# Attention, routing and two feed-forward layers in one kernel: the third batch's routing moved a round forward, and the steps at the hand-over reordered

## The reference

```python
def _attn_ref(q, k, v, alpha):           # 4 batches, 8 heads, 768 steps, head size 48
    for t in range(S):
        state = alpha[:, :, t, :, None] * state + np.einsum('bhd,bhe->bhde', k[:, :, t], v[:, :, t])
        y[:, :, t] = np.einsum('bhd,bhde->bhe', q[:, :, t], state)
def _moe_ref(x, expert_emb, tau, w1, w2):    # x: 3072 tokens of 384, 8 experts, hidden size 1024
    xn = x / (np.linalg.norm(x, axis=-1, keepdims=True) + 1e-06)
    logits = xn @ en.T / tau                 # en: the embeddings, normed alike
    expert_idx = np.argmax(logits, axis=1)
    gate_w = probs[np.arange(N), expert_idx] # probs: softmax of the logits
    for e in range(E):
        h = np.maximum(x[mask] @ w1[e], 0.0)
        out[mask] = gate_w[mask, None] * (h @ w2[e])
def _moe2_ref(x, w_in, w_out):               # hidden size 2048
    h = x @ w_in
    g = np.where(h > 0.0, h, np.exp(np.minimum(h, 0.0)) - 1.0)
    return g @ w_out
```

## Time and profile before

| | |
|---|---|
| median of 3 runs | 923.85 us (922.24 to 924.01) |
| the profiled execution | 922.87 us |
| its span | 921.2 us |
| PE busy | 886.1 us, 96% of the span |
| DVE busy | 435.5 us, 47% |
| ACT busy | 321.7 us, 35% |
| POOL busy | 273.0 us, 30% |
| mean granted clock of PE | 0.987 |

### The profile page before, as it was taken

The page is one execution under the profiler, slowest core; times in us unless marked ns, Lnnn a source line. Parts: engine busy times, 40 slices in busy tenths (PEclk is TensorE's granted clock), DMA queues, the critical chain, the costliest instruction groups (busy, mean ns, idle before and its releaser), DMA issues. The chain is left out here.

```text
span 921.2 us, 16309 instructions
## 1 busy us (share of the span) xinstructions
PE 886.1 (96%) x5729; PEld 779.3 (85%) x5729; DVE 435.5 (47%) x837; ACT 321.7 (35%) x708; POOL 273.0 (30%) x277
## 2 busy tenths in 40 slices
PE   7999999968999999999998999999999999999995
PEld 4777788757989899898997899999999999989994
DVE  6788787863222322223224545445445445445442
ACT  3556656622222222223222223223233223323221
POOL 2212444643576555635816400101001001001001
PEclk8999999979999999999999999999999999999998
DMA  9877875558768797775815301001001001000000
GB/s 151 122 132 120 167 134 107 202 176 274 267 210 283 241 336 251 203 239 150 249 32 163 121 1 44 26 1 52 18 1 61 9 0 66 4 1 35 1 1 34
DMA packets 140975, 107.92 MB, mean 117 GB/s; under 512 B 103354, under 2 KB 129074, under 8 KB 140898
## 3 DMA queue, kind: packets, MB, share of 16 engines
q0 software_dynamic: 25696, 66.09, 22.7%
q1 hardware_dynamic: 115202, 40.79, 21.1%
HBM read 89.51 MB, written 17.35 MB: 116 GB/s over the span
## 5 line engine op out<-in xcount | busy, mean ns | idle before, releaser
L1379 POOL DMA_INDIRECT out<-of,idi x24 | 23.6, 984 | 370.2 <-DVE of L1465 305.5
L1199 PE MATMUL bank<-WX,hdTh 128*128 (+1 forms) x496 | 129.0, 341 | 2.8 <-DVE hdTl L1252 1.6
L1423 PE MATMUL bank<-xT_h,wi_h 128*128 128x512 f32 x288 | 114.1, 396 | 0.0
L1423 PE MATMUL bank<-xT_l,wi_h 128*128 128x512 f32 x288 | 113.6, 394 | 0.0
L1423 PE MATMUL bank<-xT_h,wi_l 128*128 128x512 f32 x288 | 113.3, 394 | 0.0
L1483 ACT ACTIVATE ee<-bank 128x512 f32<-128x512 f32 x96 | 57.5, 598 | 147.3 <-PE bank L1423 144.5
L1505 DVE TENSOR_SCALAR em<-ee 128x512 f32<-128x512 f32 x96 | 44.4, 462 | 136.4 <-ACT ee L1483 134.3
L1120 POOL TENSOR_TENSOR WX<-raw_w,WX 128x3072 fp32r<-128x3072 f32 x14 | 95.7, 6833 | 27.7 <-DMA WX<-moe_w 19.6
L1185 PE MATMUL bank<-WX,xdTh 128*128 (+1 forms) x372 | 100.8, 407 | 1.8 <-issue 1.2
L1486 ACT ACTIVATE g_h<-gg 128x512 fp32r<-128x512 f32 x96 | 60.6, 631 | 116.0 <-DVE gg L1510 114.2
L1514 DVE TENSOR_TENSOR g_l<-gg,g_h 128x512 fp32r<-128x512 f32 x96 | 69.7, 727 | 60.2 <-ACT g_h L1486 59.3
(11 more groups left out here) (210 smaller groups left out, 1449.5 us busy)
## 6 DMA issues: line engine op xcount, KB each, us to landing
WX<-moe_w POOLq DMA_DIRECT2D x14, 1536.0 KB, 10.6
raw_w<-moe_w POOLq DMA_DIRECT2D x14, 1536.0 KB, 8.7
xd<-sorted_x SPq DMA_DIRECT2D x31, 193.0 KB, 6.7
sorted_y<-yd SPq DMA_DIRECT2D x31, 192.5 KB, 4.5
xg<-sorted_y SPq DMA_DIRECT2D x6, 770.0 KB, 4.4
nat_a<-alpha SPq DMA_DIRECT2D x32, 144.0 KB, 3.2
nat_k<-k SPq DMA_DIRECT2D x32, 144.0 KB, 3.2
nat_q<-q SPq DMA_DIRECT2D x32, 144.0 KB
```

What stands on the lines that cost most here:

```text
L1199: last = pe.matmul(y_out(t)[:, 0:DM], hdT[a][:, k * P:(k + 1) * P], WX[:, bass.ds(off + (b * WE + KD * F + k * DM), DM)], start=(k == 0 an ...
L1423: last = pe.matmul(bank[4 + i % 2][:, :], a[:, k, w], b[:, k, :], start=(k == 0 and m == 0), stop=(k == KD - 1 and m == 2))
```

## The change

For the third batch (`SOON`) `CT` moves from round 13 to the end of round 12; `Rc`, `Rb`, `Ro` from round 13 to round 12; the count steps to the start of round 13 and the choice `Y0` to `Y7` in front of `F`; the gates `Ng` to `Nr` and `Gq` from round 14 to round 13. Its norms stand in one piece ahead of `M1` in round 13, and three of its six scatters in round 13, three in round 14. On PE the transposes of the first two tiles stand together, ahead of `M10u` and the last batch's `CT`. `NM` moves ahead of `W1`; `W4` moves behind `Ro` of the last batch, where `W5` stood, and `W5` behind `Nr`. `U0` is removed: the upper half is loaded in `po_experts`, behind the third tile's arrival.

```diff
-        SOON = ({"LA": ("Rl", "Rx", "Dl")}, {"R": ("Rc", "Rb", "Ro"), "F": ("Rs",), "LA": ("Rn", "Rd", "Y0", "Y1", "Y2", "Y3", "Y4", "Y5", "Y6", "Y7"), "Qh1": ("Rw", "Rp", "Rr")},
-                {"R": ("Ng", "Nk"), "S5": ("Ns", "Nt", "Nr")})
+        SOON = ({"LA": ("Rl", "Rx", "Dl", "Rc", "Rb", "Ro")},
+                {"G": ("Rs", "Rn", "Rw", "Rd"), "S5": ("Y0", "Y1", "Y2", "Y3", "Y4", "Y5", "Y6", "Y7"),
+                 "LA": ("Ng", "Nk"), "Qh1": ("Rp", "Rr", "Ns", "Nt", "Nr")})
...
-                out_ += [("W1", 0), ("NM", PARTIAL), ("W3", 0), ("W4", 0)]
+                out_ += [("NM", PARTIAL), ("W1", 0), ("W3", 0)]
...
                 elif b == PARTIAL - 1 and r == 1:
                     i = place_of(out_, "M1")
-                    out_[i + 1:i + 1] = roots[2:]
-                    out_[i:i] = roots[:2]
-                    out_ += [(f"X{i}", b) for i in range(X_STEPS)]
+                    out_[i:i] = roots
+                    out_ += [(f"X{i}", b) for i in range(X_STEPS)] + [("SC", b * C + j) for j in range(HC)]
                 elif b == PARTIAL - 1 and r == 2:
-                    out_ += [("SC", b * C + j) for j in range(C)]
+                    i = place_of(out_, "M1") + 1
+                    out_[i:i] = [("SC", b * C + j) for j in range(HC, C)]
...
-            if n == PAIRS - 1:
-                out_.append(("U0", 1))
...
-                        d(("XT", 0), ("M10u", 0))
+                        d(("XT", 0), ("XT", 1), ("M10u", 0))
...
+            po.wait_ge(s_w, 2)
+            po.wait_ge(s_xd[EARLY], 16)
             e = expert_at(po, 1)
             for x in range(2):
-                po.wait_ge(s_w, 1 + x)
                 if x:
-                    upper_load(po, 1, e, x)
-                else:
-                    po.wait_ge(s_xd[EARLY], 16)
+                    po.wait_ge(s_raw[0], 16)
+                upper_load(po, 1, e, x)
                 raw_load(po, e, x, s_raw)
```

More of the change, by code:

```diff
@@ L290, in build @@
                 {"R": ("Rp", "Rr"), "S5": ("Ng", "Nk"), "LA": ("Ns", "Nt", "Nr")})
-        SOON = ({"LA": ("Rl", "Rx", "Dl")}, {"R": ("Rc", "Rb", "Ro"), "F": ("Rs",), "LA": ("Rn", "Rd", "Y0", "Y1", "Y2", "Y3", "Y4", "Y5", "Y6", "Y7"), "Qh1": ("Rw", "Rp", "Rr")},
-                {"R": ("Ng", "Nk"), "S5": ("Ns", "Nt", "Nr")})
-        LAST = ({"LA": ("Rl", "Rx", "Dl", "N0", "Rc", "Rb", "Ro", "W5", "Rs", "Rn", "Rd", "Rw", "Rp", "Rr", "Rz", "Ng", "Nk", "Ns", "Nt", "Nr", "W6")},)
+        SOON = ({"LA": ("Rl", "Rx", "Dl", "Rc", "Rb", "Ro")},
+                {"G": ("Rs", "Rn", "Rw", "Rd"), "S5": ("Y0", "Y1", "Y2", "Y3", "Y4", "Y5", "Y6", "Y7"),
+                 "LA": ("Ng", "Nk"), "Qh1": ("Rp", "Rr", "Ns", "Nt", "Nr")})
+        LAST = ({"LA": ("Rl", "Rx", "Dl", "N0", "Rc", "Rb", "Ro", "W4", "Rs", "Rn", "Rd", "Rw", "Rp", "Rr", "Rz", "Ng", "Nk", "Ns", "Nt", "Nr",
+                        "W5", "W6")},)
         ROUTE_VE = [SLOW] * (BATCHES - 2) + [SOON, LAST]
-        ROUTE_PE = [({}, {"Ta0": ("CT",)})] * (BATCHES - 1) + [({"YN1": ("CT",)},)]
-        ROUTE_AC = [({}, {}, {"Ln0": ("Gq",)})] * (BATCHES - 2) + [({}, {}, {"Ln0": ("Gq",)}), ({"Ln1": ("SL", "Gq")},)]
+        ROUTE_PE = [({}, {"Ta0": ("CT",)})] * (BATCHES - 2) + [({"Ys1": ("CT",)},)] + [({"YN1": ("CT",)},)]
+        ROUTE_AC = [({}, {}, {"Ln0": ("Gq",)})] * (BATCHES - 2) + [({}, {"yT0": ("Gq",)}), ({"Ln1": ("SL", "Gq")},)]
         ROUTE_PO = [({"Zm": ("ID",)},)] * BATCHES
@@ L327, in steps_ve @@
                 out_.insert(place_of(out_, "LA"), ("W0", 0))
-                out_ += [("W1", 0), ("NM", PARTIAL), ("W3", 0), ("W4", 0)]
+                out_ += [("NM", PARTIAL), ("W1", 0), ("W3", 0)]
                 out_.insert(place_of(out_, "M0") + 1, ("W2", 0))
-            if n == PAIRS - 2:
-                out_.remove(("M0", n))
-                out_.insert(0, ("M0", n))
+            if n >= PAIRS - 3:
+                m0 = ("M0", n)
+                if m0 in out_:
+                    out_.remove(m0)
+                    out_.insert(0 if n > PAIRS - 3 else place_of(out_, "Kh0"), m0)
             return out_
@@ L348, in steps_ac @@
                     out_ += [("SS", b * C + j) for j in range(4)]
+                elif r == 1 and b == PARTIAL - 1:
+                    for j, name in ((4, "Kt0"), (5, "Kt1")):
+                        out_.insert(place_of(out_, name) + 1, ("SS", b * C + j))
                 elif r == 1 and b < PARTIAL:
@@ L386, in build @@
         acA = Order(sem("acA"), [x for n in ROUNDS for x in steps_ac(n)])
-        poA = Order(sem("poA"), [x for n in ROUNDS for x in steps_po(n) if x[0] not in ("SC", "U0")])
+        poA = Order(sem("poA"), [x for n in ROUNDS for x in steps_po(n) if x[0] != "SC"])
         peD = Each({x: sem(f"peD_{x}") for x in ("HT0", "HT1", "M10", "M11", "XT", "M2")})
@@ L607, in step @@
                     for b in range(BATCHES):
-                        if n == round_of(b, 2):
+                        if n == round_of(b, 2 if b < PARTIAL - 1 else 1):
                             veA.wait(pe, "Rw", b)
@@ L661, in step @@
                     veA.wait(pe, "Ro", n)
-                    acA.wait(pe, "St5", round_of(n, 1) if n < PARTIAL else PAIRS - 1)
+                    acA.wait(pe, "St5", min(round_of(n, 1 if n < PARTIAL - 1 else 0), PAIRS - 1))
                     for x, lhsT in enumerate((before, ones)):
@@ L955, in step @@
                 u = n % 2
[L956 to L959, removed]
                 if name[0] == "X":
@@ L999, in po_a @@
                         step(name, p).then_inc(s_scat[p // C], 16)
-                    elif name == "U0":
-                        step(name, p)
                     else:
@@ L1570, in _ @@
             pe_a(pe, d)
-            d(("XT", 1), ("M10", 0), ("M11", 0), ("M10", 1), ("HT0", 0), ("HT1", 0))
+            d(("M10", 0), ("M11", 0), ("M10", 1), ("HT0", 0), ("HT1", 0))
             d(("M11", 1), ("M2", 0), ("HT0", 1), ("HT1", 1), ("M2", 1), ("XT", 2))
```

## The result

| | before | after |
|---|---|---|
| median, measured side by side (10 runs each) | 922.81 us | 924.85 us |
| lowest to highest | 921.62 to 924.22 | 922.53 to 926.64 |
| the profiled execution, its span | 922.87, 921.2 | 923.34, 921.7 |
| PE busy | 886.1 | 887.3 |
| mean granted clock of PE | 0.987 | 0.986 |

The ratio of after to before is 1.0017, with an interval of 1.0009 to 1.0025: 1.6 us slower (the two medians lie 2.0 apart), inside the 0.2% of "no change". The forecast was 3.5 us faster; the time lies above the range. The forecast of 920.3 started from the median of three runs of before, 923.85; the ten runs have theirs at 922.81, so counted from there the miss is 1.0 larger. A second measurement on another chip gave 1.0021 (1.0007 to 1.0036).

What follows compares the result with a forecast made beforehand. The fifth tile's start at 233.72 was taken as the bound, held by VectorE's chain and the second expert's weights. Freed at 230.2, it starts 3.5 us earlier: 923.85 - 3.5 = 920.3 us, range 917.1 to 923.4.

Steps and rivals of the forecast that it cites:

- The first tiles: TensorE after attention: third batch's scatters issued sooner, tiles there by about 182, ahead of 184.07; the 7.02 us wait goes.
- what was late next was VectorE: Last batch on VectorE: counts ready before VectorE can take them; read at 188.9 in place of 196.31, 7.4 us earlier.
- The weights of the second expert: GpSimd: early half no longer loaded; raw half lands at 221.2, subtraction frees the fifth tile at 230.2, TensorE waits 2.4 us.
- the forecast's fifth tile: TensorE's first product of the fifth tile starts at 230.2, 3.5 us earlier than 233.72.
- What works against it: First expert's raw weights land later, as three scatters share the DMA engines: +0.6 us taken, bounds -0.5 and +1.9.
- The pair's landing: Second expert's two loads on GpSimd: the raw half, second of two, lands 11.6 us behind its issue, at 221.2.
- Rival C: TensorE's clock falls at idle stretches ahead of the first M2 and fifth tile, costing 2.9 us: 923.2; chance 14%.
- Rival D: Raw half lands 15.1 us or more behind issue on GpSimd, undoing the gain; with 17.1 the kernel takes 925.9; chance 7%.
- B: Second expert's pair lands in 8.0 us, so VectorE's chain decides the fifth tile: 5.95 us earlier, 917.9; chance 24%.
- E: Third batch's scatters are held up and first tiles come late as before; loss and gain about cancel: 923.5; chance 8%.
- The weighed rules: Skill's load fit (9.2 us for two), set aside for the trace; VectorE-GpSimd port sharing, up to 0.8 us worse if it holds.

Runs made afterwards that it cites:

- u0_back: Changed kernel with the second expert's early half load put back at the end of GpSimd's round 15, old load order: 924.92 us beside 926.74 for before, ratio 0.9981.
- scat_late: Changed kernel with all six scatters of the third batch in round 14, none in round 13: ratio to before 1.0015.
- fill: Changed kernel with unused matmuls where TensorE idles, 11 ahead of the last pair's KT1 and 17 ahead of the fifth tile: 924.12 us, ratio to before 1.0014.
- u0_gated: As u0_back, but GpSimd issues the early load only once the first half of the first expert's raw weights has landed: ratio to before 0.9982.
- behind: Changed kernel with the early load between the last batch's norms and scatters, after raw weights and first two tiles arrive: 926.46 us beside 926.51, ratio 0.9998.
- gated_late: Changed kernel with the edits of u0_gated and scat_late joined: 921.55 us beside 923.18 for before, ratio 0.9976.
- behind_late: As behind, with all six scatters of the third batch in round 14: 925.09 us beside 926.51 for before, ratio 0.9981.

## Why the prediction was wrong

In short: the first tiles' wait went as forecast, but the first expert's raw weights landed later than the forecast allowed, and this passed through VectorE's chain, the zero rows and the second expert's loads to the fifth tile, where it used up the whole gain. The clock, which the forecast had set aside as a rival, then cost about another microsecond.

Right, by its own steps:
- *The first tiles* came in time, the 7.02 us went, and what was late next was VectorE.
- From the choice to the counts: forecast 1.45, measured 1.46. From the counts to the lower hidden part: 0.85 more than the 8.67 of before makes 9.52, measured 9.35. From the counts to the third tile's request: unchanged, 15.46 and 15.41. From there to the first load with the register behind the wait: 3.8 forecast, 3.83 measured.
- *The weights of the second expert* hold the fifth tile, and GpSimd's subtraction releases it, with 2.97 us of wait for 2.4. u0_back, which has no such wait, shows the cause.

Wrong were sizes. From the forecast's fifth tile (230.2, which is 79.68 behind the `Dl`) to the measured 83.34 are 3.7 us:
- *What works against it*, the raw weights' landing: I took +0.6, "partly in idle DMA time"; W2 came 2.37 later, over the upper bound of 1.9. This is the step that failed. The engines were at a share of 1.03 already, and in the window of 165 to 170 at 0.87: some 0.65 us of idle time, no more. The bytes were too few as well. Before, three scatters (171.61, 174.19 and 175.45) already stood beside the second of the two loads; in after all six are issued by 174.09, and the scatters' queue moves 1.18 MB up to W2, where it moved 0.38. The 0.8 MB between them are 2.1 us at 390 GB/s, an estimate near the 2.37; scat_late, which puts the scatters back, measured 1.7 to 1.9 of it. The two lines are the scatters' queue from the raw weights' request to W2, before (164.72 to 176.50) and after (164.05 to 178.10):

```profile
q0 software_dynamic: 123, 0.38, 8.6%
q0 software_dynamic: 381, 1.18, 21.8%
```

The load that `W2` waits for, the second, took 13.6 us to land, for 11.3 before. The mean of the two is 10.8, for 9.0, by the issues of the stretch from 162 to 180, in after:

```profile
raw_w<-moe_w SPq DMA_DIRECT2D x2, 1536.0 KB, 10.8
```

- The same landing went down a second way, which I had not followed: ScalarE makes the upper part of the other matrix (`Wc`, 2.77 us) ahead of the copies that TensorE needs in the last pair. It started at 172.12 behind a wait of 1.83 for the raw weights (before: 0.45), TensorE then waited 1.82, and its clock fell for 6.83 us. The last pair's rows came late to ScalarE's `last_sq`, and VectorE's `NM`, which the change moves ahead of `W1` and `W3`, waited 0.94 for it with all parts queued behind. From W2 to the choice it was 12.16 instead of 10.89, 1.27 more. It is lost between the start of `W0` (182.09) and that of `NM`: 3.03 us, for 1.78 in fill, where the clock is up, and also 1.78 in u0_back and u0_gated, where it is down for 6.83 and 3.41 us; in these three `NM` doesn't wait, and the way from W2 to the choice is 10.91. So the wait for `last_sq` is what costs, and how much of it is the clock and how much ScalarE's late start is not separated. These two, the landing and the second way, make the counts 3.04 later than forecast (42.03 for 38.99). ScalarE in after:

```profile
172.12 2.77 ACT L861 ACTIVATE WX<-raw_w 128x3072 fp32r<-128x3072 f32 x1 [1.83 <-DMA raw_w<-moe_w]
...
184.41 0.68 ACT L853 ACTIVATE last_sq<-xb 128x576 f32<-128x576 f32 x1
```

- The pair's landing: from the raw load's issue to GpSimd going on it was 12.5 us, for 11.6: +0.9 (11.9 to 12.6 in the five kernels that load this pair). The issues behind it took 1.8 for 2.2: -0.4.

Together 3.04 + 0.9 - 0.4 and 0.1 at the end of the subtraction: the 3.7, but for rounding. The gain of 3.5 at the fifth tile was gone, which comes at 83.34 for 83.20 before; a further 1.1 us is lost behind it (688.6 to the end, for 687.5).

*Rival C*, the clock, was set as a case by itself. It came on top: at the fifth tile, which C had named, and in the last pair of attention, which it had not; by its own sign, a lower clock in a stretch of 190 to 240, it happened. I had written that the prediction would be wrong at its root if TensorE lost time ahead of 184, or behind 233; it did both. Behind the fifth tile the spell of 3.41 us costs 1.55 (11.11 to the sixth tile for 9.56), where C had 2.9 for one of 5.89. *Rival D* had the right condition, raw half in late enough to undo the gain, for the most part by the wrong mechanism: the raw load was asked for later (62.10 behind the `Dl`, where the forecast had 59.1) and took 0.9 longer to be in, not 5.5. *B* and *E* did not happen: the first is refuted by the 12.5 us, the second by the tiles in time.

*The weighed rules.* The Trainium skill's fit in "DMA: Bandwidth & Descriptors", section "Anatomy of one DMA", gave an estimate of 9.2 us for the pair; the trace disagrees, with the 12.5 above, as it did for the load alone (8.0 for 5.6). Its rule in "SBUF — State Buffer", section "Who interferes with whom", was weighed on a row that doesn't carry it: the last batch's first scatter starts at 195.81, 0.82 behind its gates (194.99), just when the first part `W` ends; but the third batch's starts 0.80 behind its gates too (164.37 for 163.57), and there VectorE stood idle for 0.64 of it. The scatter's length is what fits the rule. Issued beside the second part, which ends at 196.69, it takes 1.87 and ends 0.99 behind it, where later ones take 0.96 to 1.15; in behind it is issued at 200.19 beside a part that ends at 200.73, takes 1.50 and ends 0.96 behind it. The same section infers that VectorE's work on two tensors does not hold up the descriptors of a DMA; these rows speak against that, without a run that tests it alone. At the third tile's request nothing of it is left (15.41 from the counts, for 15.46).

What stays open: why 2 us at the counts are not in scat_late's ratio; whether gated_late's lead over u0_back, u0_gated and behind_late is real, since they were measured on different chips and their intervals overlap; how the cost of taking the early load out divides between the load and the order of the others; and what the clock costs by itself in the last pair, for which ten to twelve runs of each kernel are too coarse.

## What to carry to other kernels

Don't count on idle time beside a large load that somebody waits for: read the DMA share of the stretch, and where it is at 1.0, as here, charge whatever is moved there with its full bytes, to every engine that waits for the load and not only to the one in the sum. Count the bytes up to the landing in both kernels; here the difference was 0.8 MB and not the 0.6 MB of the steps that were moved on paper. An early load that looks idle in a profile may be what keeps a chain of two loads from standing in front of a later tile; measure its removal alone (here 5.3 us, with the order of loads that came with it) before it is bundled with steps that gain. And a load that is moved goes on colliding: at three places this one cost the raw weights, the first tiles or the third tile, and no place was shown to be better than the one it had.

## What the runs showed of the hardware

- A wait of 1.82 us, with one of 0.47 behind it, was followed by 6.83 us at the lower clock, from 0.78 us behind the end of the longer one; waits of 1.72 and 1.02 us later on, at 201.98 and 208.28, left it at 1.00. So the length of a wait did not decide it alone. In the last pair the clock fell in all eight kernels in which TensorE waited 0.72 to 1.82 us at `KT1`, and in none of the five in which it waited at most 0.38 or was kept busy with extra products.
- A spell of 3.41 us at the lower clock at the fifth tile made the way to the sixth 1.55 us longer (11.11 for 9.56), where TensorE had work all the time; to the end of the kernel 1.1 of it were left.
- Of two loads of 1536 KB that SyncE issued together the second landed after 11.3 us with three scatters of 198 KB issued while they were in flight, and after 13.6 us with all six.
- With one load of 1536 KB in flight the way from the counts to the third tile's request, through eight writes of 193 KB and six scatters, took 19.9 to 20.2 us, for 15.4 to 17.0 without it.
- A scatter that GpSimd issued while VectorE worked on two tensors in SBUF ended 0.96 and 0.99 us behind the end of VectorE's instruction; the later ones, beside short instructions, took 0.96 to 1.15.
